# An explicit order for every operation on its engine, in a fused linear-attention and Fourier-mix kernel on one core

## The chip, the core and the metric

The kernel runs on one core of a Trainium2 chip. The metric is the device time of one execution in microseconds (us). The core has five engines with instruction queues of their own, which the profile names PE (TensorE, with PEld for its weight loads), DVE (VectorE), ACT (ScalarE), POOL (GpSimd) and SP (SyncE, which only issues transfers here). Each engine works through its queue in order, and queues wait for each other by semaphores.

## The reference, cut to what matters

Four batches, eight heads, 768 steps of time, 48 channels per head. The first part is a linear attention with a decaying state, the second a Fourier mix and an MLP of 384 to 1536 to 384:

```python
for t in range(S):
    cur = np.einsum('bhd,bhe->bhde', u[None] * kt, vt)
    y[:, :, t] = np.einsum('bhd,bhde->bhe', rt, state + cur)
    state = wt[:, :, :, None] * state + np.einsum('bhd,bhe->bhde', kt, vt)
...
X = np.fft.fft(np.fft.fft(x, axis=1), axis=2)
u = x + np.real(X)
un = (u - mu) / np.sqrt(var + 1e-06)
out = u + np.maximum(un @ w_ch1, 0.0) @ w_ch2
```

## The kernel before

The time axis is cut into chunks of 128 steps: 6 chunks per batch, 24 in all, numbered n. `attention(b, c)` describes one chunk. The logarithm of the decay (`Ln`, tile lb) is summed along time by two matmuls (`tce`, `tci`), exponentials on ScalarE (`ex`, `ew`) make the decays, VectorE and GpSimd multiply them onto r and k (`rh`, `kh`), TensorE transposes both (`trr`, `trk`), the copies `rT` and `kT` bring the transposes from PSUM to SBUF, `am` makes the matrix of scores, VectorE masks it (`ms`, tile ah), `sm` and `st` carry the state on, and `y` makes the result; `rk`, `rku`, `dc`, `vtd` and `yx` add the term with u. In batch 0 `kh` is VectorE's, later GpSimd's, behind the exponential of line 736 (tile e). `fe` and `fo` fold the result for the Fourier sums.

`mix(b)` does the rest of a batch: `sq` (sequence sums, matmuls of 193 columns), `hc` and `hr` (copies), `dm` (sums over the channels), `uf`, `bs`, `ba` (residual, mean and variance), `un`, `tr`, `ut` (normalised, transposed, copied out of PSUM), then layer 1 (`m1`, line 958) with its relu (`rl`) and layer 2 (`m2`, line 974) with `ob` (tile osb) and the transfer out. Before all that, set-up makes the tables of sines and cosines: VectorE computes arguments (line 553 writes them), ScalarE takes sines, loads its table of logarithm and exponential (line 640), VectorE mirrors the tables and TensorE rearranges them (line 679). Unused columns of some tiles are filled with zeros once (line 556).

No loop order decides when an operation runs. Every operation is registered with `op` under a kind and a number, with its engine, its planned duration and what it reads and writes. `schedule` then plays the plan through: at each step it takes, over all engines, the ready operation that can start first, ties broken by the number in `PLAN`, with limits on open PSUM tiles per pool (`caps`: 5 for attention, 4 for the mix, 1 for the fillers). What comes out is a fixed queue per engine. `PLACES` holds a digit for each operation that can run on two engines: 0 ScalarE, 1 VectorE for `rT`, `kT`, `hc`, `ut` and `rl`. Loads keep the order w, k, r, v of each chunk (`o.prev`). `fill_gaps` puts matmuls of zeros, the fillers of line 1015, where the plan leaves TensorE idle, from the first operation `beat` until planned time 56 us; they keep one PSUM bank.

```python
c = (s, o.key, o.idx)
if best is None or c < best[0]:
    best = (c, o)
```

Of the kernel before, what the change touches and what calls it, by code (L numbers as in the profile page):

```python
# [7 lines left out]
ALU = mybir.AluOpType  # L8
# [24 lines left out]
class _Prog:  # L33
# [13 lines left out]
    RATE = 192.0  # L47
    AHEAD = 1500.0
    DMA_LEAD = 500.0

    def __init__(self, nc, caps, plan, places):
        self.nc = nc
        self.ops = []
        self.wr = {}
        self.rd = {}
        self.caps = caps
        self.plan = plan
        self.places = places

# [3 lines left out]
    def op(self, lab, alts, r=(), w=(), sem=None, nbytes=0, fix=0.0):  # L63


        kind, n = lab
# [31 lines left out]
    def schedule(self):  # L98
        free = [0.0] * 8
        users = [()] * 8  # L100
        BUSY = 1e17
        held = {p: 0 for p in self.caps}
        engt = {e: 0.0 for e in self.ENGS}
        avail = {e: [] for e in self.ENGS}
        order = {e: [] for e in self.ENGS}
        dma_t = 0.0
        port_t = 0.0
        for o in self.ops:
            for d in o.deps:
                d.users.append(o)  # L110
            o.nd = len(o.deps)
            o.ready = o.ready0
            if o.nd == 0:
                avail[o.eng].append(o)
        left = len(self.ops)
        while left:
            best = None
            spare = sorted(f for f in free if f < BUSY)
            for e in self.ENGS:
                for o in avail[e]:  # L120
                    if o.prev is not None and o.prev.start is None:
                        continue
                    s = max(engt[e], o.ready)
                    if o.port:
                        s = max(s, port_t)
                    if o.bytes and e == "sp":
                        s = max(s, dma_t - self.AHEAD)
                    if o.opens:
                        new = [x for x in o.tile if x.ops[0] is o]
                        if held[new[0].pool] + len(new) > self.caps[new[0].pool] or len(spare) < len(new):  # L130
                            continue
                        s = max(s, spare[len(new) - 1])
                    c = (s, o.key, o.idx)
                    if best is None or c < best[0]:
                        best = (c, o)
# [3 lines left out]
            avail[e].remove(o)  # L139
            for x in o.tile:  # L140
                if x.ops[0] is o:
                    idle = [i for i in range(8) if free[i] <= s]
                    if idle:
                        x.bank = max(idle, key=lambda i: (free[i ^ 1], -i))
                    else:
                        x.bank = min(range(8), key=lambda i: (free[i], i))
                    o.deps.update(users[x.bank])
                    free[x.bank] = BUSY
                    held[x.pool] += 1
# [9 lines left out]
            order[e].append(o)  # L159
            for x in o.tile:  # L160
                x.n_done += 1
                x.end = max(x.end, o.end)
                if x.n_done == len(x.ops):
                    held[x.pool] -= 1
                    free[x.bank] = x.end + self.BANK_LAT
                    users[x.bank] = tuple(x.ops)
            for u in o.users:
                if o.bytes:
                    t = o.end
                elif e == u.eng == "pe":  # L170
                    t = engt[e]
                else:
                    t = o.end + self.LAT[e][u.eng]
                u.ready = max(u.ready, t)
                u.nd -= 1
                if u.nd == 0:
                    avail[u.eng].append(u)
# [4 lines left out]
    def fill_gaps(self, fn, tile, dur, spare, until):  # L182
# [5 lines left out]
        for o in self.order["pe"]:  # L188
            n = int((o.start - t - spare) // dur) if first.start < o.start <= min(until, last.start) else 0
# [105 lines left out]
    def _topo(self):  # L295
# [3 lines left out]
        while n < len(self.ops):  # L299
# [13 lines left out]

PLAN = {
    "set": [573, -700, -711, -727, -138, 1123, 29, -1164, 314, 1326, 325, -916, -2410, -588, -1687, -469, 1954, -296, 3463,
# [4 lines left out]
    "zero": [2203],  # L320
    "load": [2835, -3063, -2612, -1806, 887, -2150, 635, -954, 767, 394, 1084, -1028, -1889, -641, -923, 248, -88, -1448,
           2009, -1694, -1788, 966, -1289, -1158],
    "Ln": [284, -611, 1645, -1456, -2505, 255, -669, 148, 585, -1351, -1052, -503, -1122, 769, 337, 3689, -172, -915, 688,
           -3266, 412, 3417, -623, -5688],
    "tce": [-1829, -3214, -1237, -1827, -876, 33, -456, -1340, -1828, -2352, 144, 733, -77, -51, -421, 1795, -245, -547, -113,
           -1271, 702, 1074, -434, 693],
    "tci": [1561, -9, -2535, 1234, -298, 3695, -2840, -1446, -1807, -1864, 1253, -2594, 653, -665, -434, -773, 1708, -5099,
           748, -2106, 1377, -22, 669, 128],
    "ex": [-3131, 1004, -188, 739, 237, 1443, -1155, 5815, -1424, -194, 2886, -202, 469, 929, 431, -3017, -1192, -640, -1072,
           -655, 2635, -532, -275, -1379],  # L330
    "tot": [-105, -660, -616, 1383, -1284, 0, -2541, -1074, -1853, -911, -928, 0, 1115, -2238, 147, -601, 792, 0, 96, -1156,
           203, -267, -1607],
# [9 lines left out]
    "vtd": [2161, -2040, -532, -1785, -2577, 377, -865, 1608, 3126, 1151, 2646, -927, 358, -1231, -1689, -3886, -971, -1826,
           -95, -3035, -391, 789, -1252, 795],
    "vb": [-955, -2112, 3388, 415, -509, -390, -277, 132, -715, 1212, 427, 4272, -590, 346, -2779, 390, 792, 158, 2849, 907,
           1735, 830, 58, 3257],
    "rh": [412, 1151, -212, 2002, 243, 179, 159, 1558, -530, -1849, -1998, -751, -415, -500, 247, -1541, 471, 1405, -2535,
           -1777, -1851, -220, 556, -1131],
# [84 lines left out]
def bass_rwkv6_finch__then__fnet_fourier_mix_kernel(  # L432
# [13 lines left out]
    CH = 128  # L446
# [603 lines left out]
```

How the kernel before makes its waits and increments, by code:

```python
        def run(name, eng):  # L259
            for o in self.order[name]:
                for c, v, d in sorted(o.waits, key=lambda x: x[2].end):
                    eng.wait_ge(sems[c], d.val)
                ins = o.fn(eng)
                if o.sem is not None:
                    ins.then_inc(sems[o.sem], 16)
                elif o.inc:
                    ins.then_inc(sems[name], 1)
            if name == "dve":
                for s in dcount:
                    if s.startswith("out"):
                        eng.wait_ge(sems[s], dcount[s])
                eng.nop()
```

## Time and profile before

| | |
|---|---|
| median of 3 runs | 204.85 us (204.56 to 205.8) |
| the profiled execution | 204.85 us, its span 203.1 us |
| TensorE | 190.9 us busy, 1847 matmuls |
| VectorE | 170.4 us busy, 430 instructions |
| ScalarE | 126.6 us busy |
| GpSimd | 109.5 us busy |

The span runs from the first to the last instruction of the profiled execution; the rest of its time lies around that. A busy time is the union of an engine's instruction records. Matmuls are pipelined, so that records of neighbours overlap. "Idle before" is the time for which an engine had nothing in work ahead of an instruction, with what released it.

### The profile page before, as it was taken

How to read it: one execution, taken by the hardware profiler on the slowest of the kernel's cores; microseconds unless marked ns; L12 is line 12 of the kernel's file. 1: busy time of each engine (PE TensorE's matmuls, PEld its weight loads, DVE VectorE, ACT ScalarE, POOL GpSimd, SP SyncE). 2: the span in 40 equal slices, each digit the busy share in tenths (PEclk: the TensorE clock that was granted, in tenths of full speed). 3: DMA queues.
4: the chain of work that ended last, by engine and by line, in shares of the span. 5: the costliest groups of instructions: out<-in, count | busy, mean ns of one | idle time of the engine just before them, and what ended most of it. 6: DMA issues, size and time to landing. Idle time of an engine off the chain costs nothing.

```text
span 203.1 us, 4857 instructions
## 1 busy us (share of the span) xinstructions
PE 190.9 (94%) x1847; PEld 124.0 (61%) x1847; DVE 170.4 (84%) x430; ACT 126.6 (62%) x291; POOL 109.5 (54%) x131
## 2 busy tenths in 40 slices
PE   0999899999999999899899999999999999999993
PEld 0765575766656666666456667666666666666561
DVE  8939997989889899999999999998989769674332
ACT  4589785336757989667989587549872452936000
POOL 2353759741038899999699789992233550000000
PEclk9999999999999999999999999999999999999999
DMA  6999998999999707999999659512001200210033
GB/s 129 193 202 195 198 204 140 200 184 185 195 187 206 160 0 160 215 186 199 268 175 226 137 136 211 122 39 81 0 3 39 81 0 0 84 37 0 0 116 116
DMA packets 105414, 26.45 MB, mean 130 GB/s; under 512 B 100272, under 2 KB 105008, under 8 KB 105392
## 3 DMA queue, kind: packets, MB, share of 16 engines
q1 hardware_dynamic: 103440, 23.80, 55.2%
q0 software_dynamic: 1952, 2.36, 7.0%
q8 instruction: 14, 0.23, 0.4%
q14 instruction: 8, 0.07, 0.1%
HBM read 23.79 MB, written 4.72 MB: 140 GB/s over the span
## 4 chain that ended last, share of the span: by engine, by line
PE 63%; DVE 22%; POOL 7%; ACT 3%; issue 3%; POOLq 0%; DVEq 0%; ACTq 0%
PE bank L958 19%; PE bank L974 19%; PE bank L1015 5%; DVE ah L796 4%; PE bank L887 4%; PE bank L913 3%; POOL rk L545 2%; PE bank L791 2%; DVE st L817 2%; DVE uf L918 2%; POOL kh L545 2%; DVE rh L753 2%; PE bank L931 2%; PE bank L769 2%; DVE bst L921 2%
## 5 line engine op out<-in xcount | busy, mean ns | idle before, releaser
L958 PE MATMUL bank<-unt,w 128*128 128x384 bf16 x288 | 54.2, 326 | 0.8 <-ACT ht L963 0.3
L974 PE MATMUL bank<-w,ht 128*128 128x384 bf16 x288 | 52.5, 326 | 0.3 <-ACT ht L963 0.2
L963 ACT ACTIVATE ht<-bank 128x384 bf16<-128x384 f32 x59 | 28.5, 492 | 13.6 <-PE bank L958 13.3
L974 PEld LDWEIGHTS bank<-w,ht 128*128 128x128 bf16 x288 | 26.6, 98 | 16.2 <-ACT ht L963 0.4
L958 PEld LDWEIGHTS bank<-unt,w 128*128 128x128 bf16 x288 | 25.9, 97 | 16.6 <-ACT ht L963 0.7
L796 DVE TENSOR_TENSOR ah<-bank,msk 128x512 bf16<-128x512 f32 x48 | 31.3, 679 | 1.5 <-PE bank L791 1.3
L545 POOL TENSOR_TENSOR vtd<-in_v,dc 128x384 f32<-128x384 f32 x24 | 19.9, 829 | 18.4 <-DVE dc L744 12.7
L545 POOL TENSOR_TENSOR kh<-in_k,e 128x384 bf16<-128x384 f32 x18 | 18.0, 1002 | 16.3 <-ACT e L736 16.3
L545 POOL TENSOR_TENSOR rk<-in_r,in_k 128x384 f32<-128x384 f32 x24 | 23.9, 1000 | 4.9 <-DMA in_r<-in_r_dram 4.8
L964 DVE TENSOR_SCALAR ht<-bank 128x384 bf16<-128x384 f32 x37 | 19.7, 552 | 7.6 <-PE bank L958 7.4
L545 POOL TENSOR_TENSOR rk<-rk,ub 128x384 f32<-128x384 f32 x24 | 23.9, 999 | 2.5 <-DMA ub<-in_u_dram 1.8
L559 ACT ACTIVATE un<-uf,agg 128x384 bf16<-128x384 f32 x24 | 14.1, 609 | 15.6 <-DVE agg L923 15.4
L980 DVE SCALAR_TENSOR_TENSOR osb<-bank,rstd,uf 128x384 f32<-128x384 f32 x24 | 14.4, 609 | 11.0 <-PE bank L974 10.2
L545 POOL TENSOR_TENSOR xf<-fd,ft 128x384 bf16<-128x384 f32 x18 | 17.7, 1001 | 9.4 <-DVE ft L859 8.4
L1015 PE MATMUL bank<-wz 128*128 128x256 bf16 x105 | 16.6, 297 | 4.8 <-DVE wz L556 4.8
L846 ACT ACTIVATE x<-bank 128x384 f32<-128x384 f32 x24 | 11.8, 490 | 9.8 <-DVE bank L842 5.4
L721 ACT ACTIVATE bank<-bank 128x384 f32<-128x384 f32 x24 | 11.8, 491 | 8.5 <-PE bank L715 8.5
L753 DVE TENSOR_TENSOR rh<-bank,in_r 128x384 bf16<-128x384 f32 x24 | 13.2, 549 | 3.3 <-ACT bank L721 3.2
L817 DVE TENSOR_TENSOR st<-bank,e 64x192 bf16<-64x192 f32 x40 | 14.0, 351 | 1.4 <-PE bank L835 0.8
L1015 PEld LDWEIGHTS bank<-wz 128*128 128x128 bf16 x105 | 10.7, 106 | 7.2 <-DVE wz L556 4.8
L744 DVE TENSOR_REDUCE dc<-rk 128x8 f32<-128x384 f32 x24 | 12.9, 541 | 0.1
L918 DVE TENSOR_TENSOR uf<-bank,x 128x384 f32<-128x384 f32 x24 | 12.6, 545 | 0.2 <-PE bank L913 0.2
(120 smaller groups left out, 373.0 us busy)
## 6 DMA issues: line engine op xcount, KB each, us to landing
in_w<-in_w_dram SPq DMA_DIRECT2D x24, 192.0 KB, 3.9
in_k<-in_k_dram SPq DMA_DIRECT2D x24, 192.0 KB, 4.0
in_r<-in_r_dram SPq DMA_DIRECT2D x24, 192.0 KB, 4.2
in_v<-in_v_dram SPq DMA_DIRECT2D x24, 192.0 KB, 4.0
out_dram<-osb SPq DMA_DIRECT2D x24, 192.0 KB, 1.9
w<-in_moe_w_ch_dram POOLq DMA_DIRECT2D x2, 1152.0 KB, 13.7
ub<-in_u_dram SPq DMA_DIRECT2D x1, 192.0 KB, 4.4
```

The source lines that it names most:

```text
L545: return shared(lambda e: e.tensor_tensor(out=o, in0=a, in1=b, op=f))
L559: return lambda e: e.activation(o, a, f, **kw)
L753: op(("rh", n), ("dve", 551, lambda e: e.tensor_tensor(out=rh[:, :, 0:D], in0=ps(tce)[:, 0:DM].rearrange("t (h d) -> t h d", d=D), in1=rt[ ...
L796: masked[n] = op(("ms", 2 * n + x), ("dve", 682, lambda e, x=x: e.tensor_tensor(out=ah[:, x:H:2, :], in0=ps(ta[x])[:, :].rearrange("p (h t ...
L817: op(("st", 2 * n + x), ("dve", 360, lambda e, x=x, pr=pr: e.tensor_tensor(out=s_out[pr, :, D * x:D * x + D], in0=ps(tds)[pr, 0:DM].rearra ...
L918: op(("uf", n), ("dve", 543, lambda e, kb=kb, t=t: e.tensor_tensor(out=uf[:, kb, :], in0=ps(t)[:, 0:DM], in1=xb[:, kb, 0:DM], op=ALU.add)) ...
L958: ins = e.matmul(ps(t)[:, 0:384], W1[:, m, 128 * j:128 * j + 128], unt[:, m, :], start=(m == 0), stop=(m == NM - 1))
L963: ("act", 490, lambda e, j=j, t=t, ht=ht: e.activation(ht[:, j, :], ps(t)[:, 0:384], ACTF.Relu)),
L964: ("dve", 552, lambda e, j=j, t=t, ht=ht: e.tensor_scalar(out=ht[:, j, :], in0=ps(t)[:, 0:384], scalar1=0.0, scalar2=None, op0=ALU.max))],
L974: ins = e.matmul(ps(t)[:, 0:DM], ht[:, j, 128 * x:128 * x + 128], W2[:, j, :], start=(j == 0), stop=(j == NJ - 1))
L980: op(("ob", n), ("dve", 614, lambda e, kb=kb, t=t, o=o: e.scalar_tensor_tensor(out=o[:, :], in0=ps(t)[:, 0:DM], scalar=rstd[:, kb:kb + 1], ...
L1015: return e.matmul(ps(tw)[:, 0:256], WZ[:, 0:128], WZ[:, :])
```

## The change

The numbers in `PLAN` become places: `schedule` sorts each engine's operations by them and takes only the head of each queue. Its planned times now set nothing but the PSUM bank of a tile and the number of fillers. The limits per pool and the fixed order of loads are gone, and so is the wait of `tce` for the mask of two chunks before. Set-up registers index patterns and fills first, then the tables; a fill may be VectorE's or GpSimd's by a digit in `PLACES`, and two state fills become one. `sq` places pairs of matmuls together. The second `beat`, where the fillers end, now reads what a relu of the first half batch writes. A few planned durations and rates differ.

```diff
-    def __init__(self, nc, caps, plan, places):
+    def __init__(self, nc, plan, places):
...
     def schedule(self):
+        order = {e: sorted((o for o in self.ops if o.eng == e), key=lambda o: o.key) for e in self.ENGS}
+        head = {e: 0 for e in self.ENGS}
...
-            for e in self.ENGS:
-                for o in avail[e]:
-                    if o.prev is not None and o.prev.start is None:
+            for x, e in enumerate(self.ENGS):
+                if head[e] >= len(order[e]):
+                    continue
+                o = order[e][head[e]]
+                if o.nd:
+                    continue
...
-    "zero": [2203],
+    "zero": [51, 7, 15, 8, 11, 38, 40, 42, 3, 2, 10, 15, 9, 50, 5, 46, 4, 8, 18, 41, 6, 7, 1],
...
-    "beat": [-514, 2562],
+    "beat": [113, 118],
...
 PLACES = {
-    "rT": "010000010000010000110111",
-    "kT": "110011011000100111000100",
-    "hc": "110001010000",
-    "ut": "011111000001000010010101",
-    "rl": "101111100000001000000010101000000001000011111000010000100000100110110100111111010010100001111000",
+    "zero": "01011000011100000010100",
+    "rT": "100000110100000010000100",
+    "kT": "010000011100000010011000",
+    "hc": "001000000001",
+    "ut": "100100000000000000000101",
+    "rl": "011100001100010011010000100000100000010000000110000110011001100000101011010000000111010101110010",
 }
...
+    def zeros(ap, dve, pool, w, val=0.0):
+        f = fill(ap, val)
+        op(("zero", 0), [("dve", dve + 35, f), ("pool", pool, f)], w=w)
...
         for i in range(2):
-            put("dve", 145, fill(ST[i][0:64, :, D:2 * D], 0.0), w=[("ST", i, 0)])
-            put("dve", 145, fill(ST[i][64:128, :, 0:D], 0.0), w=[("ST", i, 1)])
+            zeros(ST[i][:, :, :], 223, 480, [("ST", i, 0), ("ST", i, 1)])
...
-        if n >= 2:
-            o.deps.add(masked[n - 2])
...
-    small_constants()
+    iotas()
+    fills()
     tables()
     masks()
-    fills()
     mirrors()
...
-    for i in range(2):
-        o = op(("beat", i), ("pe", 110, beat), r=["WZ"], w=[tw])
-        o.ready0 = WARM * i
+    op(("beat", 0), ("pe", 110, beat), r=["WZ"], w=[tw])
+    op(("beat", 1), ("pe", 110, beat), r=["WARM"], w=[tw])
     g.schedule()
-    g.fill_gaps(beat, tw, 110.0, 150.0, WARM)
+    g.fill_gaps(beat, tw, 110.0, 150.0)
```

TensorE's queue from its start. Lines 1015 and 989 are fillers, 679 and 652 the tables, 715 and 686 `tce`, 719 and 688 `tci`, 725 and 694 `tot`, lb0 and lb1 the logarithms of chunks 0 and 1. Before:

```order
L1015 MATMUL bank0<-wz 128x256 x37
L679 MATMUL bank1<-ss,nidw 128x193
L679 MATMUL bank1<-cs,rev 128x193
L679 MATMUL bank1<-ss,idw 128x191
L679 MATMUL bank1<-cs,rev 128x191
L679 MATMUL bank2<-cs,rev 128x193
L679 MATMUL bank2<-cs,rev 128x191
L679 MATMUL bank3<-ss,nidw 128x193 x2
L679 MATMUL bank3<-ss,idw 128x191 x2
L715 MATMUL bank4<-lb0,msk 128x384
L719 MATMUL bank5<-lb0,nle 128x384
L725 MATMUL bank5<-one,lb0 128x1 x4
```

After:

```order
L652 MATMUL bank0<-ss,nidw 128x193
L652 MATMUL bank0<-cs,rev 128x193
L652 MATMUL bank0<-ss,idw 128x191
L652 MATMUL bank0<-cs,rev 128x191
L652 MATMUL bank1<-cs,rev 128x193
L652 MATMUL bank1<-cs,rev 128x191
L688 MATMUL bank2<-lb1,nle 128x384
L694 MATMUL bank2<-one,lb1 128x1 x4
L652 MATMUL bank3<-ss,nidw 128x193 x2
L652 MATMUL bank3<-ss,idw 128x191 x2
L686 MATMUL bank4<-lb0,msk 128x384
L686 MATMUL bank5<-lb1,msk 128x384
```

The 37 fillers ahead of the tables are gone, and chunk 1's sums stand among the tables. The queue after has a filler in two places only, both amid layer 1 of the first half batch.

VectorE's queue in set-up, where the first steps of the tables stand (ht1 and uf1 are scratch; the first rows before are the end of the fills that begin the queue). Before, the ninth instruction to the first table step:

```order
L556 MEMSET kh0 128x8x8
L556 MEMSET kh2 128x8x8
L556 MEMSET bhpi 128x1
L556 MEMSET lb1 128x8x8
L556 MEMSET beps 128x1
L556 MEMSET xf0 128x6x32
L556 MEMSET lb0 128x256
L550 TENSOR_SCALAR chs<-tc 128x1
L549 TENSOR_SCALAR tn<-tc 128x3
L549 TENSOR_SCALAR msk<-ht1 128x128
L549 TENSOR_SCALAR sgi<-tci 128x1
L550 TENSOR_SCALAR ht1<-ht1,tn 128x194
```

After, the first twelve:

```order
L517 TENSOR_SCALAR tn<-tc 128x3
L524 MEMSET ss 128x3
L517 TENSOR_SCALAR msk<-ht1 128x128
L524 MEMSET kh1 128x8x8
L524 MEMSET xf0 128x6x33
L524 MEMSET st1 128x192
L518 TENSOR_SCALAR ht1<-ht1,tn 128x194
L524 MEMSET cs 128x3
L524 MEMSET x0 128x6x4
L524 MEMSET lb2 128x8x8
L518 TENSOR_SCALAR nle<-ht1 128x128
L518 TENSOR_SCALAR ht1<-ht1 128x194
```

The first step of the tables (`ht1<-ht1,tn`) moves from twentieth to seventh place.

ScalarE's queue where batch 0 reaches the MLP: un is the normalised row, ht the relu, e_1 the exponential on which GpSimd's `kh` of chunk 7 waits. Before:

```order
L559 ACTIVATE un<-uf,agg 128x384
L963 ACTIVATE ht<-bank 128x384
L559 ACTIVATE un<-uf,agg 128x384
L944 ACTIVATE lnv<-agg,beps 128x3
L963 ACTIVATE ht<-bank 128x384
L559 ACTIVATE vb<-in_v 128x384
L947 ACTIVATE rstd<-lnv 128x3
L559 ACTIVATE lb<-in_w 128x8x48
L963 ACTIVATE ht<-bank 128x384
L846 ACTIVATE x<-bank 128x384
L736 ACTIVATE e_1<-bank 128x388
L721 ACTIVATE bank<-bank 128x384
```

After:

```order
L750 ACTIVATE ktb<-bank 128x512
L875 ACTIVATE hcs<-bank 128x2x193 x2
L527 ACTIVATE vb<-in_v 128x384
L527 ACTIVATE un<-uf,agg 128x384 x3
L914 ACTIVATE unt<-bank 128x3x128 x2
L690 ACTIVATE bank<-bank 128x384
L705 ACTIVATE e_1<-bank 128x388
L527 ACTIVATE lb<-in_w 128x8x48
L527 ACTIVATE un<-uf,agg 128x384
L938 ACTIVATE ht<-bank 128x384 x2
L914 ACTIVATE unt<-bank 128x3x128
L938 ACTIVATE ht<-bank 128x384 x2
```

That exponential has moved ahead of the first relu; before, it stood behind four.

The order of the loads changes too: r2, k0, r1, w0, u, w1, k1, r0, w2, w3, r3, k2, v0 are the first thirteen (the digit is the chunk), in place of w0, k0, r0, v0, u, w1, k1, r1, v1, w2, k2, r2, v2.

## Rows read from the trace of the kernel before

**Rows 1.** The page: span, then part 1, busy time, share, instructions.
```profile
span 203.1 us, 4857 instructions
...
PE 190.9 (94%) x1847; PEld 124.0 (61%) x1847; DVE 170.4 (84%) x430; ACT 126.6 (62%) x291; POOL 109.5 (54%) x131
```

**Rows 2.** Stages: length, then busy (x instructions) PE, PEld, DVE, ACT, POOL; clock, DMA.
```profile
10.80:49.80 39.00, 37.03 (x407) 24.47 (x407) 33.02 (x78) 25.18 (x62) 22.69 (x26) 1.00 1.07 191
49.80:140.00 90.20, 87.96 (x926) 57.21 (x927) 85.05 (x200) 68.26 (x158) 72.62 (x81) 1.00 0.77 162
140.00:200.00 60.00, 59.92 (x485) 37.85 (x481) 41.99 (x97) 27.59 (x64) 10.89 (x13) 1.00 0.10 37
```

**Rows 3.** The same view of L1015 alone: PE, PEld; clock, DMA; two calls.
```profile
0.00:10.80 10.80, 5.98 (x37) 4.46 (x37) 1.00 0.81 163
10.80:49.80 39.00, 10.31 (x68) 6.15 (x67) 1.00 1.07 191
...
7.80:8.80 1.00, 1.00 (x7) 0.76 (x6) 1.00 0.93 187
8.80:9.80 1.00, 1.00 (x11) 0.90 (x10) 1.00 1.09 214
```

**Rows 4.** Timeline of PE: start, us, instruction.
```profile
10.78 0.26 PE L679 MATMUL bank<-ss,nidw 64*128 64x193 bf16 x1
```

**Rows 5.** Timeline of DVE, set-up; in brackets the idle time before.
```profile
2.76 0.31 DVE L550 TENSOR_SCALAR ht<-ht,tn 128x194 f32<-128x194 f32 x1
...
5.55 1.16 DVE L553 SCALAR_TENSOR_TENSOR uf<-ht,tc 128x194 f32<-128x194 f32 x1
...
7.50 0.40 DVE L553 SCALAR_TENSOR_TENSOR uf<-ht,tc 128x194 f32<-128x194 f32 x1
...
8.02 0.34 DVE L553 SCALAR_TENSOR_TENSOR ht<-uf 128x194 f32<-128x194 f32 x1
...
13.08 0.56 DVE L753 TENSOR_TENSOR rh<-bank,in_r 128x384 bf16<-128x384 f32 x1 [2.29 <-ACT bank L721]
```

**Rows 6.** Timeline of ACT, set-up.
```profile
8.94 1.28 ACT L640 ACT_TABLE_LOAD   x1
...
10.66 0.51 ACT L559 ACTIVATE lb<-in_w 128x384 bf16<-128x384 f32 x1
```

**Rows 7.** Timeline of POOL, set-up and batch 0 to 1.
```profile
5.50 1.00 POOL L545 TENSOR_TENSOR rk<-in_r,in_k 128x384 f32<-128x384 f32 x1 [3.55 <-DMA in_r<-in_r_dram]
8.29 1.00 POOL L545 TENSOR_TENSOR rk<-rk,ub 128x384 f32<-128x384 f32 x1 [1.80 <-DMA ub<-in_u_dram]
...
31.46 0.93 POOL L690 DMA_DIRECT2D w<-in_moe_w_ch_dram  x1
...
58.05 1.01 POOL L545 TENSOR_TENSOR kh<-in_k,e 128x384 bf16<-128x384 f32 x1 [10.90 <-ACT e L736]
```

**Rows 8.** Timeline of SP, the queue that issues the loads (fifth and thirteenth).
```profile
3.73 0.71 SPq L580 DMA_DIRECT2D ub<-in_u_dram  x1
...
11.62 0.90 SPq L575 DMA_DIRECT2D in_v<-in_v_dram  x1
```

**Rows 9.** The chain that ended last: start, us, what.
```profile
29.57 0.65 PE bank L824 x2
...
49.81 3.59 PE bank L958 x21
...
69.91 0.82 POOL vtd L545
...
177.98 10.24 PE bank L958 x63
```

**Rows 10.** Groups of DVE by form: busy us, mean ns of one, idle before.
```profile
L940 DVE CAST unt<-bank 128x384 bf16<-128x384 f32 x10 | 5.4, 547 | 0.0
L782 DVE COPY ktb<-bank 128x512 bf16<-128x512 bf16 x11 | 4.6, 416 | 0.3 <-PE bank L775 0.3
...
L901 DVE CAST hcs<-bank 128x386 bf16<-128x386 f32 x4 | 2.2, 588 | 0.6 <-PE bank L887 0.6
```

More of the change, by code:

```diff
@@ L55, in __init__ @@
         self.rd = {}
-        self.caps = caps
         self.plan = plan
         self.places = places
+        self.count = {}
     def tile(self, pool):
@@ L63, in op @@
     def op(self, lab, alts, r=(), w=(), sem=None, nbytes=0, fix=0.0):
-        kind, n = lab
+        kind = lab[0]
+        n = self.count.get(kind, 0)
+        self.count[kind] = n + 1
         if isinstance(alts, tuple):
@@ L98, in schedule @@
     def schedule(self):
+        order = {e: sorted((o for o in self.ops if o.eng == e), key=lambda o: o.key) for e in self.ENGS}
+        head = {e: 0 for e in self.ENGS}
+        engt = {e: 0.0 for e in self.ENGS}
+        BUSY = 1e17
         free = [0.0] * 8
         users = [()] * 8
[L101 to L105, printed above, removed]
         dma_t = 0.0
@@ L117, in schedule @@
             best = None
-            spare = sorted(f for f in free if f < BUSY)
-            for e in self.ENGS:
-                for o in avail[e]:
-                    if o.prev is not None and o.prev.start is None:
-                        continue
[L123 to L135, printed above, removed]
+            for x, e in enumerate(self.ENGS):
[4 more added lines that the diff above has]
+                    continue
+                s = max(engt[e], o.ready)
+                if o.opens:
+                    n = sum(t.ops[0] is o for t in o.tile)
+                    spare = sorted(f for f in free if f < BUSY)
+                    if len(spare) < n:
+                        continue
+                    s = max(s, spare[n - 1])
+                a = s
+                if o.bytes and e == "sp":
+                    s = max(s, dma_t - self.AHEAD)
+                if o.port:
+                    s = max(s, port_t)
+                if best is None or (s, a, x) < best[0]:
+                    best = ((s, a, x), o)
             assert best is not None, "no operation can start"
@@ L138, in schedule @@
             e = o.eng
-            avail[e].remove(o)
-            for x in o.tile:
-                if x.ops[0] is o:
+            head[e] += 1
+            for t in o.tile:
+                if t.ops[0] is o:
                     idle = [i for i in range(8) if free[i] <= s]
[L143 to L149, printed above, removed]
+                    t.bank = max(idle, key=lambda i: (free[i ^ 1], -i))
+                    o.deps.update(users[t.bank])
+                    free[t.bank] = BUSY
             o.start = s
@@ L158, in schedule @@
                 o.end = s + o.dur + (self.DRAIN if e == "pe" else 0.0)
[L159 to L166, printed above, removed]
+            for t in o.tile:
+                t.n_done += 1
+                t.end = max(t.end, o.end)
+                if t.n_done == len(t.ops):
+                    free[t.bank] = t.end + self.BANK_LAT
+                    users[t.bank] = tuple(t.ops)
             for u in o.users:
@@ L188, in fill_gaps @@
         for o in self.order["pe"]:
-            n = int((o.start - t - spare) // dur) if first.start < o.start <= min(until, last.start) else 0
+            n = int((o.start - t - spare) // dur) if first.start < o.start <= last.start else 0
             for i in range(n):
@@ L342 @@
[L342 to L347, printed above, removed]
@@ new lines @@
+    "beat": [113, 118],
[23 rows of a table added]
+    "zero": [51, 7, 15, 8, 11, 38, 40, 42, 3, 2, 10, 15, 9, 50, 5, 46, 4, 8, 18, 41, 6, 7, 1],
[19 rows of a table added]
+    "rku": [13, 14, 17, 21, 27, 28, 34, 44, 43, 49, 57, 52, 63, 77, 83, 85, 82, 91, 96, 99, 112, 118, 117, 121],
+    "vtd": [20, 22, 23, 24, 29, 31, 37, 46, 50, 54, 60, 58, 70, 78, 86, 88, 90, 97, 109, 104, 119, 122, 124, 127],
+    "wgt": [30, 40],
[3 rows of a table added]
+    "load": [3, 1, 7, 12, 4, 5, 6, 2, 16, 8, 11, 0, 15, 9, 13, 10, 20, 14, 22, 18, 25, 17, 21, 19, 28, 23, 24, 29, 26, 27, 32,
[3 rows of a table added]
@@ L647, in mirrors @@
             lo = [(n + "l", q) for q in range(NS)]
-            put("dve", 60, fill(T[:, :, 1, HK - 1:HK], 0.0), w=[(n + "x", q) for q in range(NS)])
             put("dve", 303, ts(T[:, :, 0, HQ:HK], T[:, :, 0, HQ - 2::-1], sg[:, :], None, ALU.mult),
```

152 lines of the change are left out of this document (64 added, 88 removed), and 129 rows, old and new, of the table PLAN.

## The prediction

> **What bounds the kernel now.** I read the busy shares first, then the span by stage, and only then single waits, because the shares mislead here. TensorE shows 94% busy and VectorE 84% [rows 1]. By stage [rows 2] VectorE is busy 33.0 of the 39.0 us from 10.8 to 49.8 us and 85.1 of the 90.2 us up to 140 us (94%); after that it falls to 42.0 of 60.0, while TensorE is busy throughout. So VectorE sets the pace until about 140 us, and TensorE the rest. TensorE's 98% in the middle stage overstates it: records of matmuls overlap, and 63 matmuls of 384 columns really take 10.24 us, 163 ns each [rows 9].
>
> Part of TensorE's busy time is no work at all: fillers (matmuls of zeros, L1015) take 5.98 us before 10.8 us and 10.31 us of the stage behind it [rows 3]. Real work starts at 10.78 us because the tables aren't there earlier [rows 4]. VectorE makes their arguments, and its first product of the attention (rh) starts at 13.08 us after an idle 2.29 us [rows 5]. The chain to there: the last argument at 8.02 us on VectorE [rows 5], ScalarE's sine of it, the table load at 8.94 us, the logarithm (lb) at 10.66 us [rows 6]. The MLP's first layer (L958) starts at 49.81 us [rows 9].
>
> **The change part by part.** All sums go against the profiled execution: 204.85 us, of which 203.1 us is the span [rows 1] and 1.75 us lies around it. The median of the runs shown is the same 204.85.
>
> *Set-up, -2.0 us.* Before, fifteen fills stand ahead of the tables on VectorE and the first table step starts at 2.76 us [rows 5]. Now two small set-up steps and four fills do, and it can start near 2.1 us: 0.65 us. Between first and last argument fills, sign columns and the second identity leave (about 1.2 us of start-to-start time) and four small ones come (0.5 us): 0.7 us. One step took 1.16 us, its sister 0.40 [rows 5]: it ran beside GpSimd's rk of 5.50 us [rows 7]. That rk now waits for k1, the seventh load, and stays clear: 0.76 us. So the last argument comes 2.1 us earlier and the table load ends near 8.1 us. There the loads become the limit, w1 being the sixth now. The fifth (ub), issued at 3.73 us [rows 8], had landed by 8.29 us [rows 7]; from it to the thirteenth issue at 11.62 us [rows 8] it is 0.99 us a load, so w1 lands near 9.2 us. Then a logarithm of 0.51 [rows 6], a matmul and its wait, about 0.35, and two exponentials in a queue on ScalarE, about 0.9: rh at about 11.0 instead of 13.08 us. Bounds: -3 us (w1 comes sooner) to +1 us (GpSimd's fills are slow and loads late). The v0 load falls from fourth to thirteenth place: 11.62 + 4.56 (ub's time) = 16.2 us. TensorE's queue holds its first reader, the state matmul, and what stands behind that; VectorE has ten other operations until then. I count 0, at worst 1 us.
>
> The eight fills on GpSimd lie in its idle 3.55 us ahead of rk [rows 7]: 0, at worst half a microsecond for those ahead of the tables' index pattern.
> The Trainium skill speaks against it: "SBUF — State Buffer", section "Who interferes with whom", says that GpSimd and VectorE share a port pair, and that a tensor_scalar in a two-port mode and a GpSimd operation shut each other out. By that a fill beside a table step can hold it up; with half a microsecond for it (an estimate) the whole would be 199.9 us. The 1.16 us row agrees that the two collide; no run here shows a GpSimd fill doing it.
>
> *Batch 0, -2.5 us.* Copies out of PSUM move from VectorE to ScalarE: in batch 0 three kT, one hc and three ut leave, one relu comes. At 416, 588 and 547 ns [rows 10], the relu priced as ut, that is 1.25 + 0.59 + 1.64 - 0.55 = 2.9 us; neighbours overlap by some 0.08 us each, so 2.5. VectorE's idle time in 10.8 to 49.8 us is 6.0 us, 2.3 of it the wait for the first rh, so 3.7 us of slack: I count all of the 2.5. Bounds: -4 (waits shrink too) to 0 (ScalarE, busy 25.2 of 39.0 us [rows 2], answers later).
>
> *Batches 1 and 2, -2.5 us.* Two hc, two ut, two kT and one relu leave VectorE, two rT come: 1.18 + 1.09 + 0.83 + 0.55 - 0.83 = 2.8 us, net 2.4, in the stage where VectorE is 94% busy. By its records TensorE can give only 2.2 us there, by its spacing more. A second effect: GpSimd idled 10.90 us until 58.05 us, waiting for the exponential e [rows 7], and from 69.91 us it carries the longest chain [rows 9]. The changed order puts that exponential ahead of the MLP's first relu, so kh comes some 10 us earlier. I count 2.5 us for both, between 0 (TensorE full) and 5. Batch 3's moves lie where TensorE sets the pace: 0. W1's transfer stood behind vtd of chunk 4, issued at 31.46 us [rows 7], and still does: 0. W2 now stands behind kh of chunk 7; most of layer 1 covers it; if not, up to 3 us.
>
> *Fillers, +1.5 us.* 103 of 105 go; the two left stand inside layer 1. Fillers number 7 in the microsecond from 7.8 us and 11 in the next [rows 3]: TensorE goes from its lower level, 1.2 GHz, to 2.4 GHz there, after some four microseconds of fillers back to back, though the column of the granted clock prints 1.00. Now the tables meet a TensorE that has done nothing. One chunk's chain through it is 2688 columns (1.14 us at 163 ns per 384) and yx, 0.65 [rows 9]: 1.8 us, at the low level as much again. I take 1.5 for the first chunk, as the wait for v0 hides a little. Bounds: -1.5 us (a filler of 0.11 us less ahead of some dozen real matmuls) to the first rival.
> The skill's page "TensorE: Matmul & The Clock Gate", Part 1, says that the slow level is the default and that activity releases it; the rows above agree. By it batch 0 begins slowly and stays so while TensorE does little, which is the first rival.
>
> Sum: -2.0 - 2.5 - 2.5 + 1.5 = -5.5; 204.85 - 5.5 = 199.35, so **199.4 us**. The tail, one osb and its transfer behind the last matmul, stays.
>
> **The rivals.** (A, slower) *TensorE stays at 1.2 GHz through batch 0.* For: before, only fillers are seen to raise the clock. Against: at half speed the work is twice as dense. Price: per chunk 4352 columns (1.84 us) and yx 0.65, times six 15.0; sequence mixing 48 x 193 columns 3.9, model mixing 18 x 0.163 = 2.9, transposes 0.5: 22.3 us. Doubled, begun at 8.8 us, and with 3.7 us of waits it ends at 57.1, 7.3 us behind 49.81: 204.85 + 7.3 - 2.5 = **209.7 us**. It is slower than before once more than about 17.5 of the 22.3 us run low.
> (B, no change) *GpSimd holds the middle.* For: it is busy 72.6 of 90.2 us [rows 2], carries the chain from 70 us, and its work is the same. Then head and batch 0 only wait in front of it, the fillers' cost is hidden with them, and batches 1 and 2 give 1.2: **203.7 us**. Against: its idle 10.9 us just before. That *the order doesn't do what it says* belongs here: it is frozen from planned times, and if loads land 2 us later than counted, TensorE stands at v0 with all behind it and the head's gain is gone twice: 199.4 + 2.0 + 2.0 = 203.4.
> (C, much faster) *The clock costs nothing and GpSimd's early start pays in full:* 204.85 - 2.0 - 2.5 - 5.0 = **195.4 us**.
>
> **How the numbers follow.** Forecast 0.54, A 0.14, B with the frozen order 0.16, C 0.16. A measurement here can tell about 1%, 2 us, from no change. The forecast's own range, 197 to 202.5, and C are faster: 0.70. B, and a little of A, is within 1%, 202.8 to 206.9: 0.17. The rest of A is slower: 0.13. The range reaches past C and over half of A: 194.5 to 207.5.
>
> **What would show it.** Right: last argument near 6 us, first rh near 11, the first matmul of layer 1 near 46 to 48, kh of chunk 7 ten microseconds earlier, VectorE's total down by some 9 us, the first 384-column matmuls about 320 ns apart and soon 163. Wrong: the wide spacing into batch 0's mixing (A); an early head but the same stage from 70 us on (B); TensorE waiting for v0 or W2.

## Result and the profile after

The changed kernel takes 198.51 us (median of 4 runs, 198.09 to 199.0) against 204.81 us beside it; the ratio is 0.9685, 95% interval 0.965 to 0.9721. In a second series it took 197.97 us (6 runs) against 205.09, ratio 0.9663 (0.9636 to 0.969). So it is 6.3 to 7.1 us faster; 199.4 was forecast, with a range of 194.5 to 207.5.

The page of the changed kernel: span, busy shares, granted clock, chain by engine.

```profile
span 196.7 us, 4656 instructions
...
PE 178.9 (91%) x1744; PEld 117.1 (60%) x1744; DVE 161.9 (82%) x403; ACT 133.2 (68%) x308; POOL 110.9 (56%) x139
...
PEclk9999699999999999999999999999999999999999
...
PE 73%; DMA 7%; DVE 6%; issue 5%; POOL 4%; ACT 4%; DVEq 0%; POOLq 0%; ACTq 0%
```

Against [rows 1] VectorE has 8.5 us less to do, ScalarE 6.6 more and GpSimd 1.4 more. TensorE is busy 12 us less, though 16.3 us of fillers went [rows 3]: the fillers' records overlap those of real matmuls by 3.8 us, and the real matmuls alone cover 178.1 us before and 178.9 us after. Transfers hold 7% of the chain in this execution. In the trace of after_again (the second series) they hold none:

```profile
PE 83%; DVE 9%; ACT 4%; issue 2%; POOL 0%; DVEq 0%; POOLq 0%; ACTq 0%
```

By stage, to be read beside [rows 2] (the borders are the first table, the first matmul of layer 1, 140 us as there, and the end of TensorE's work):

```profile
8.40:46.60 38.20, 33.17 (x357) 21.82 (x357) 32.40 (x80) 29.07 (x68) 23.25 (x30) 0.96 1.00 193
46.60:140.00 93.40, 92.14 (x969) 61.16 (x965) 86.81 (x207) 74.72 (x177) 73.53 (x82) 1.00 0.81 164
140.00:193.00 53.00, 53.00 (x424) 33.97 (x423) 35.63 (x79) 24.40 (x58) 12.54 (x15) 1.00 0.11 39
```

VectorE's share in the middle is 93%, nearly what it was (94%). What fell is its rest behind 140 us, from 42.0 to 35.6 us. About 2.8 us of that (an estimate from the rows of copies) are batch 3's own copies, of which a net six went to ScalarE; most of the rest must have been done earlier.

VectorE's timeline in the set-up, and its last instruction:

```profile
2.14 0.20 DVE L518 TENSOR_SCALAR ht<-ht,tn 128x194 f32<-128x194 f32 x1
...
5.47 0.41 DVE L521 SCALAR_TENSOR_TENSOR uf<-ht,tc 128x194 f32<-128x194 f32 x1
...
6.13 0.35 DVE L521 SCALAR_TENSOR_TENSOR ht<-uf 128x194 f32<-128x194 f32 x1
...
11.92 0.56 DVE L722 TENSOR_TENSOR rh<-bank,in_r 128x384 bf16<-128x384 f32 x1 [3.50 <-ACT bank L690]
...
193.68 0.62 DVE L955 SCALAR_TENSOR_TENSOR osb<-bank,rstd,uf 128x384 f32<-128x384 f32 x1 [0.68 <-PE bank L949]
```

Before, the last instruction stood 6.34 us later:

```profile
200.02 0.62 DVE L980 SCALAR_TENSOR_TENSOR osb<-bank,rstd,uf 128x384 f32<-128x384 f32 x1 [0.68 <-PE bank L974]
```

ScalarE in the set-up:

```profile
7.07 1.28 ACT L614 ACT_TABLE_LOAD   x1
8.68 0.94 ACT L527 ACTIVATE lb<-in_w 128x384 bf16<-128x384 f32 x2 [0.32 <-DMA in_w<-in_w_dram]
...
11.31 0.47 ACT L690 ACTIVATE bank<-bank 128x384 f32<-128x384 f32 x1 [0.51 <-PE bank L686]
```

The tables' last argument comes 1.9 us earlier than in [rows 5], the step that took 1.16 us takes 0.41, and the logarithm (lb) comes 2.0 us earlier than in [rows 6]. From lb to the first rh, though, it is 3.24 us where it was 2.42, and VectorE idles 3.50 us in front of it. TensorE's timeline says why, and shows two later places:

```profile
10.75 0.85 PE L686 MATMUL bank<-lb,msk 128*128 128x384 bf16 x2
11.39 0.53 PE L688 MATMUL bank<-lb,nle 128*128 128x384 bf16 x1
...
20.49 1.49 PE L793 MATMUL bank<-vtd,ht 128*128 128x384 f32 x2
...
27.44 0.83 PE L793 MATMUL bank<-vtd,ht 128*128 128x384 f32 x2
...
46.80 0.65 PE L933 MATMUL bank<-unt,w 128*128 128x384 bf16 x3
...
61.75 0.81 PE L949 MATMUL bank<-w,ht 128*128 128x384 bf16 x4 [1.00 <-DMA w<-in_moe_w_ch_dram]
```

At 10.75 us two matmuls of 384 columns take 0.64 us from start to the next start, 320 ns each: 1.2 GHz, although the clock's column prints 1.00 there. The pair of matmuls of yx at 20.49 us is slow again, 1.49 us where a later one takes 0.83. Layer 1 begins at 46.80 us (before: 49.81 [rows 9]), and layer 2 waits 1.00 us for its weights W2 at 61.75 us. GpSimd's timeline belongs to that:

```profile
33.87 0.93 POOL L663 DMA_DIRECT2D w<-in_moe_w_ch_dram  x1
...
47.53 1.00 POOL L513 TENSOR_TENSOR kh<-in_k,e 128x384 bf16<-128x384 f32 x1 [4.10 <-ACT e L705]
48.47 1.07 POOL L664 DMA_DIRECT2D w<-in_moe_w_ch_dram  x1
```

kh of chunk 7 stands at 47.53 us in place of 58.05 [rows 7], with 4.10 us of idle time ahead of it in place of 10.90. W2 is issued behind it. VectorE's groups by form, for [rows 10]:

```profile
L751 DVE COPY ktb<-bank 128x512 bf16<-128x512 bf16 x7 | 2.9, 417 | 0.9 <-PE bank L744 0.9
L751 DVE COPY rtb<-bank 128x512 bf16<-128x512 bf16 x6 | 2.5, 411 | 0.1
L915 DVE CAST unt<-bank 128x384 bf16<-128x384 f32 x4 | 2.2, 552 | 0.8 <-PE bank L906 0.8
L876 DVE CAST hcs<-bank 128x386 bf16<-128x386 f32 x2 | 1.2, 598 | 2.1 <-PE bank L858 2.1
```

Four kT, two rT, six ut and two hc copies and three relus have left VectorE on balance; each of the copies that stayed costs what it did.

### The profile page after: what moved, and what is told of

The parts are those of the page before. It is cut to its first block, busy times and chain, and to the rows that moved or that the text cites. A ratio compares the mean times of both kernels' runs of the same rounds, so it can differ in the third digit from the quotient of the medians.

```text
span 196.7 us, 4656 instructions
## 1 busy us (share of the span) xinstructions
PE 178.9 (91%) x1744; PEld 117.1 (60%) x1744; DVE 161.9 (82%) x403; ACT 133.2 (68%) x308; POOL 110.9 (56%) x139
## 4 chain that ended last, share of the span: by engine, by line
PE 73%; DMA 7%; DVE 6%; issue 5%; POOL 4%; ACT 4%; DVEq 0%; POOLq 0%; ACTq 0%
PE bank L949 24%; PE bank L933 19%; DMA w<-in_moe_w_ch_dram 7%; PE bank L888 4%; PE bank L858 3%; PE bank L744 3%; PE bank L760 3%; PE bank L738 2%; PE bank L688 2%; PE bank L804 2%; PE bank L686 2%; PE bank L906 2%; PE bank L801 1%; PE bank L793 1%; PE bank L778 1%
## 5 line engine op out<-in xcount | busy, mean ns | idle before, releaser
L949 PE MATMUL bank<-w,ht 128*128 128x384 bf16 x288 | 55.5, 326 | 1.0 <-DMA w<-in_moe_w_ch_dram 1.0
L938 ACT ACTIVATE ht<-bank 128x384 bf16<-128x384 f32 x62 | 29.3, 492 | 17.6 <-PE bank L933 14.3
L939 DVE TENSOR_SCALAR ht<-bank 128x384 bf16<-128x384 f32 x34 | 18.3, 548 | 8.3 <-PE bank L933 8.2
L527 ACT ACTIVATE lb<-in_w 128x384 bf16<-128x384 f32 x24 | 12.5, 526 | 0.3 <-DMA in_w<-in_w_dram 0.3
L896 DVE BATCH_NORM_STATS2 bst<-uf 128x6 f32<-128x384 f32 x24 | 12.6, 545 | 0.1
```

Source lines behind the costliest of these rows:

```text
L527: return lambda e: e.activation(o, a, f, **kw)
L938: ("act", 490, lambda e, j=j, t=t, ht=ht: e.activation(ht[:, j, :], ps(t)[:, 0:384], ACTF.Relu)),
L939: ("dve", 552, lambda e, j=j, t=t, ht=ht: e.tensor_scalar(out=ht[:, j, :], in0=ps(t)[:, 0:384], scalar1=0.0, scalar2=None, op0=ALU.max))],
L949: ins = e.matmul(ps(t)[:, 0:DM], ht[:, j, 128 * x:128 * x + 128], W2[:, j, :], start=(j == 0), stop=(j == NJ - 1))
```

## Experiments

Ratios are to the kernel before, run beside each. The changed kernel stands at 0.9685 and 0.9663, so differences under about 0.7 us from it are not told apart; where a difference in us to it is given, it is (ratio - 0.967) x 205.

**The set-up.** All 23 fills on VectorE, 22 of them first:

```diff
-    "zero": [51, 7, 15, 8, 11, 38, 40, 42, 3, 2, 10, 15, 9, 50, 5, 46, 4, 8, 18, 41, 6, 7, 1],
+    "zero": [50, -30, -29, -28, -27, -26, -25, -24, -23, -22, -21, -20, -19, -18, -17, -16, -15, -14, -13, -12, -11, -10, -9],
...
-    "zero": "01011000011100000010100",
+    "zero": "00000000000000000000000",
```

> The changed kernel with all its constant fills on VectorE and 22 of them ahead of the tables, as the kernel before had it; nothing else moves. T (the head start of the set-up is kept to the end): the last table argument comes at about 8 us in place of 6.13, the first rh at 13 to 13.5, and the time rises by 1.0 to 1.9 us to 199.5 to 200.4. Rival (the start is absorbed by the first batch, whose chunks wait for other things): 198.1 to 198.9.

Measured: 199.0 us, ratio 0.9712 (0.9674 to 0.975): 0.9 us up, too near the interval to count. VectorE's timeline shows that the start moves as a whole:

```profile
7.16 0.35 DVE L521 SCALAR_TENSOR_TENSOR ht<-uf 128x194 f32<-128x194 f32 x1
...
12.92 0.56 DVE L722 TENSOR_TENSOR rh<-bank,in_r 128x384 bf16<-128x384 f32 x1 [3.55 <-ACT bank L690]
```

Last argument and first rh are both 1.0 us later than in the changed kernel (the trace is of the slowest of four runs, 200.65 us). So the places of the fills are worth 1.0 us at the head, about half of the 2.06 us that the set-up gains there when TensorE is not slow (fillers_head, below).

**The fillers.** Three kernels. The first puts 46 fillers back ahead of the tables, the second has them in TensorE's gaps as well, and the third takes 103 out of the kernel before.

```diff
# fillers_head
-    "beat": [113, 118],
+    "beat": [-2, -1],
...
-    "zero": [51, 7, 15,
+    "zero": [-1, 7, 15,
...
-    op(("beat", 1), ("pe", 110, beat), r=["WARM"], w=[tw])
+    op(("beat", 1), ("pe", 110, beat), r=["NIDW"], w=[tw])
-    g.fill_gaps(beat, tw, 110.0, 150.0)
+    g.fill_gaps(beat, tw, 165.0, 150.0)
# fillers_through: the same, but
+    "beat": [-1, 118],
...
     op(("beat", 1), ("pe", 110, beat), r=["WARM"], w=[tw])
# before_no_fillers
-    g.fill_gaps(beat, tw, 110.0, 150.0, WARM)
+    g.fill_gaps(beat, tw, 110.0, 150.0, 0.0)
```

> The changed kernel with 46 filler matmuls put back, all of them ahead of the first table matmul, as in the kernel before; nothing else moves. T (the low clock of the first chunk is a price that still stands in the new order): TensorE is at 2.4 GHz from about the first table matmul on, the tables and the first 384-column matmuls take half as long, the first rh comes at about 11.0 us in place of 11.92, there is no low stretch at 20.7 to 24.1, and the time falls by 1.0 to 1.5 us, to about 197.3. Rival (the low clock is hidden beside VectorE and ScalarE, which have the set-up to do): 198.1 to 198.9, no change. Second rival (the fillers delay the tables, being in front of them on TensorE): over 199.

> The changed kernel with fillers ahead of the tables as in fillers_head, and now also in TensorE's gaps of the first chunks, as the kernel before had them. fillers_head measured a ratio of 0.9643 against before where the changed kernel had 0.9685, and in its trace the clock was granted in full for only 6.8 us and was then at 1.2 GHz for 10.2 us, over the gap in front of chunk 0. T (that second low stretch costs about as much as the first saved): TensorE stays at 2.4 GHz from the tables on, the first rh comes at about 11.0, the first layer-1 matmul a further 0.5 to 1 us earlier than in fillers_head, and the time is 0.5 to 1.0 us under it, about 197. Rival (after the first rh the chunks wait for VectorE and GpSimd, and the clock is covered): as fillers_head, within 0.3 us.

> The kernel before with 103 of its 105 fillers left out and nothing else changed. T: it pays what the prediction put on the fillers, 1.5 us: TensorE stays at 1.2 GHz until about 17 us, the first rh comes 0.3 to 1 us later than 13.08, and the time is about 206.3. Rival (fillers are only in the way, and the low clock is hidden): 204.8 or up to 1 us less.

fillers_head: 197.84 us, 0.9643 (0.962 to 0.9665), 0.6 us down, not told apart from nothing. In its trace the first rh comes at 11.02 us, 0.90 earlier, as theory T had it; but TensorE falls back at once. Its timeline:

```profile
10.05 0.49 PE L686 MATMUL bank<-lb,msk 128*128 128x384 bf16 x2
...
13.15 1.07 PE L744 MATMUL bank<-idw,kh 128*128 128x128 bf16 x8 [2.37 <-DVE kh L726]
...
14.33 0.85 PE L688 MATMUL bank<-lb,nle 128*128 128x384 bf16 x2
```

The pair of 384-column matmuls takes 0.49 us ahead of the wait of 2.37 us and 0.85 behind it. The 0.90 us last for a while: layer 1 starts 0.93 us earlier than in the changed kernel (45.87 against 46.80).

```profile
45.87 2.11 PE L933 MATMUL bank<-unt,w 128*128 128x384 bf16 x12
```

Behind that the two executions come together. The wait for W2 is 1.4 us in this one and 1.0 in the other, and the last osb is 0.13 us earlier (193.55 against 193.68).

fillers_through: 199.05 us, 0.9708 (0.9677 to 0.974), 0.8 us up; T falls. In its trace the first table matmuls take 0.26 us each, as in fillers_head (0.34 in the changed kernel), no low stretch follows, and the first rh comes at 10.90 us. Yet nothing is gained: layer 1 starts at 47.62 us, 1.75 later than in fillers_head, where T had it earlier. ScalarE's start times, laid side by side with those of the changed kernel, are 1.28 us ahead at 14 us, 0.94 at 27, 0.18 at 32, and 0.82 behind at 46. One place can be read in TensorE's timeline: two fillers stand at 27.69 us ahead of yx, with no idle time beside them, and TensorE, 0.84 us ahead until then, is 0.43 ahead behind them. That fillers in gaps of the plan that are none in the run did the rest too is likely, but not shown place by place. As its fillers hold the queue up, this kernel can't say what a full clock alone would be worth at the end.

before_no_fillers: 1.0063 (1.0032 to 1.0094), 1.3 us slower, the size that T had; but the place seems to be another. Its twelve runs fall into three groups: four with a mean clock of 1.00 took 205.2 to 205.5 us, no more than before; five with 0.992 took 207.0 to 207.2; three with 0.982 or 0.983 took 208.1 to 208.6. The first rh comes at 13.24 us (before: 13.08). The trace is of one of the last three (208.3 us). It has a low stretch around the first matmuls of layer 1, behind three microseconds in which TensorE is busy 1.16:

```profile
47.00:50.00 3.00, 1.16 (x9) 0.58 (x9) 3.00 (x10) 1.95 (x5) 0.00 (x0) 0.83 1.26 204
50.00:53.00 3.00, 2.37 (x9) 1.19 (x9) 2.39 (x6) 1.33 (x3) 0.00 (x0) 0.50 0.97 194
```

So in the old order the fillers bought nothing at the first chunk that shows. That they paid ahead of layer 1 is what this one trace suggests; where the other runs had their low stretches is not known, so it is not shown.

**Copies against order.** 85 of the 180 copies out of PSUM (rT, kT, hc, ut and the relus) change engine, 51 from VectorE to ScalarE and 34 back: 17 net. In each of these four kernels the order is planned as it was, the copies named change engine, and every engine's list is then sorted by planned start; the other instructions keep their order, but for a filler here and there. The PSUM banks of the tiles are planned anew along with it, and what that does is not parted from what the engines do. The core of the edit in the changed kernel:

```diff
+        keep = [set(o.deps) for o in self.ops]
+        self.play({e: sorted((o for o in self.ops if o.eng == e), key=lambda o: o.key) for e in self.ENGS})
+        for o, d in zip(self.ops, keep):
...
+            if o.lab[0] in OLD:
+                o.eng, o.dur, o.fn = o.alts[int(OLD[o.lab[0]][o.idx0])]
...
+        self.play({e: sorted((o for o in self.ops if o.eng == e), key=lambda o: o.start) for e in self.ENGS})
```

> The changed kernel's order, with the rT, kT, hc, ut and rl copies put back on the engine (VectorE or ScalarE) that they had in the kernel before, each at its planned place in time; TensorE's and GpSimd's orders and the set-up stay as in the changed kernel. T (the gain behind the set-up comes from the work taken off VectorE): loses 4 to 4.5 of the 6.3 us, about 202.8, VectorE busy about 8 us more. Rival (the order alone makes the gain, and where a copy runs is worth little): within 1 us of 198.5.

> The kernel before, in its own scheduler's order, with the rT, kT, hc, ut and rl copies put on the engines that they have in the changed kernel, each at its planned place in time; set-up, fills and fillers stay as before, GpSimd's order is the same. T (work taken off VectorE is the gain): VectorE is busy some 8 us less than 170.4, and the time falls by 3 to 5 us, to about 201. Rival (the copies' engines are worth nothing without the new order): 204 to 206, no change or slightly worse, the old order being made for the old places. old_places measured the other corner: 205.8, no gain left with the new order and the old places.

> The changed kernel's order with only 17 copies put back from ScalarE to VectorE at their planned places (2 rT, 4 kT, 2 hc, 6 ut, 3 rl, spread over the program), which is the whole net shift of copies between the two engines; old_places put back all 85 that changed engine (51 one way, 34 the other) and measured 205.8. Load theory (17 copies' worth of time on VectorE is the gain): VectorE as busy as in old_places, 168, and nearly the same time, 204 to 206. Fit theory (each order is made for its own places, and each copy on the other engine costs where it stands): about 17 of the 85 misfits, a rise of 1 to 2 us over the changed kernel, 199.5 to 201.

> The kernel before in its own order with 17 copies moved from VectorE to ScalarE at their planned places (2 rT, 4 kT, 2 hc, 6 ut, 3 rl), the net shift of the change and nothing else; before_new_places, with all 85, measured 210.8. Load theory: VectorE's busy time falls by about 8 us and the time by 2 to 4 us, to 201 to 203. Fit theory: no gain, 205 to 207, the copies being late or in the way on ScalarE where they now stand.

| order | all 85 on the other kernel's engine | the net 17 alone |
|---|---|---|
| new | old_places 205.8, 1.0023 (1.0004 to 1.0042) | net_back 202.72, 0.9882 (0.9854 to 0.991) |
| old | before_new_places 210.82, 1.0275 (1.024 to 1.0309) | before_net 205.26, 1.0009 (0.9991 to 1.0027) |

Busy shares and chain of net_back:

```profile
PE 181.8 (91%) x1744; PEld 117.6 (59%) x1744; DVE 168.4 (84%) x420; ACT 126.7 (63%) x291; POOL 111.0 (55%) x139
...
PE 58%; DVE 36%; issue 3%; ACT 2%; POOL 0%; DVEq 0%; POOLq 0%; ACTq 0%
```

and of before_net:

```profile
PE 191.7 (94%) x1847; PEld 124.5 (61%) x1847; DVE 165.3 (81%) x413; ACT 133.2 (65%) x308; POOL 110.1 (54%) x131
...
PE 62%; DVE 22%; ACT 12%; issue 2%; DVEq 0%; ACTq 0%
```

with the chain of the kernel before for it:

```profile
PE 63%; DVE 22%; POOL 7%; ACT 3%; issue 3%; POOLq 0%; DVEq 0%; ACTq 0%
```

In the new order 17 copies back on VectorE give it 6.5 us more work, the end comes 4.3 us later, and VectorE's share of the chain rises from 6% or 9% (the two traces of the changed kernel) to 36%: here VectorE's load is on the path. In the old order the same shift takes 5.1 us off VectorE, gives ScalarE 6.6 us more, and the time doesn't move. With all 85, VectorE has 3.9 us less to do (166.5) and the kernel is 5.8 us slower. In the new order too the load is not all: old_places has the same 168.4 us on VectorE as net_back and is 2.9 us slower. So neither theory holds by itself. The load theory had the right direction in the new order, but forecast 204 to 206 for net_back, and it fails in the old order; the fit theory was right on before_net and priced net_back two to four times too low. Each of these kernels changes ScalarE's work by as much as VectorE's or more, so none of them parts the two; that it is VectorE's load which counts in the new order is read from the chain alone.

Part of net_back's loss may be the clock's. In its trace 384-column matmuls are slow up to 22.59 us and fast at 25.92, while in the changed kernel's trace the clock was granted in full from 17.3 to 20.7 us. Its layer 1 starts at 49.24 us, 2.44 later than in the changed kernel, from the same first rh (11.92):

```profile
22.59 0.48 PE L702 MATMUL bank<-lb,msk 128*128 128x384 bf16 x1 [0.21 <-DVE dc L729]
...
25.92 0.33 PE L704 MATMUL bank<-lb,nle 128*128 128x384 bf16 x1
...
49.24 2.11 PE L949 MATMUL bank<-unt,w 128*128 128x384 bf16 x12 [0.64 <-ACT lb L543]
```

fills_first, slow as long and with no copy moved, falls back 0.7 us against the changed kernel over the same stretch. So some 1.7 of the 2.44 us are left for the copies (an estimate).

The Trainium skill, "Perfetto Trace Analysis", section "Optimizing Scalar/DVE Operations", says that moving work to ScalarE may make sense where VectorE is saturated. VectorE looks saturated in both kernels (94% and 93% of the middle stage); net_back agrees with the page; in before_net the move gains nothing.

**GpSimd.** The kernel before, where GpSimd's product for the u-term has 128x1x2 elements from chunk 6 on (it leaves out most of that term):

```diff
-        op(("rku", n), product(rk[:, :, :], rk[:, :, :], UB[:, :, :], ALU.mult, 1000),
+        few = (slice(None), slice(0, 1 if n >= NC else H), slice(0, 2 if n >= NC else D))
+        op(("rku", n), product(rk[few], rk[few], UB[few], ALU.mult, 1000),
```

> The kernel before, in the same order on every engine, with GpSimd's product for the u-term cut to 128x1x2 elements from chunk 6 on; it leaves out most of that term in these chunks, about 16 us of GpSimd's work from 50 us on. Rival B of the prediction (GpSimd holds the middle): TensorE's waits between 60 and 140 us go and the time falls by 3 us or more, to 202 or less. T (VectorE and its share of copies hold it): falls by less than 1 us.

Measured: 205.06 us, 1.0007 (0.9984 to 1.0031). Its stage from 60 to 140 us, and below it the same of the kernel before:

```profile
60.00:140.00 80.00, 78.03 (x843) 50.88 (x842) 76.51 (x180) 61.36 (x142) 57.99 (x79) 1.00 0.74 158
```

```profile
60.00:140.00 80.00, 78.03 (x842) 50.80 (x840) 76.47 (x180) 61.41 (x142) 70.68 (x80) 1.00 0.75 160
```

GpSimd has 12.7 us less to do there, and the busy times of the other engines stay the same. So GpSimd's load does not hold the middle, though its vtd stood in the longest chain [rows 9], and rival B is out.

**W2 and the loads.**

```diff
-    "wgt": [30, 40],
+    "wgt": [30, 30.5],
```

> The changed kernel with the second weight load issued by GpSimd right behind the first, ahead of kh of chunk 6, instead of behind kh of chunk 7; all else keeps its order. T (TensorE's 1.0 us wait for these weights at 61.75 is on the path): the wait goes and the time falls by 0.5 to 1.0 us against the changed kernel. Rival (the wait is covered by the work that TensorE would wait for next, or the earlier transfer takes time from the chunk loads): within 0.3 us, or slower.

> The changed kernel itself, once more, beside head_and_w2 on the same chip, to have differences under 1 us from one chip. Every theory: 198.0 to 199.0 and a ratio of 0.966 to 0.971 to the kernel before.

w2_early: 198.75 us, 0.9683 (0.9648 to 0.9717): no gain. The 1.00 us wait is gone from its trace, and that execution took 197.62 us; but the trace of after_again, the changed kernel once more (197.69 us), has no such wait either. So the wait belongs to some executions only (fills_first has one of 1.3 us), and this pair can't say what an earlier W2 is worth where the wait occurs.

> The changed kernel with the fillers of fillers_head and the early second weight load of w2_early together, as a version that may beat both kernels. Two gains that add (0.85 us and the 1.0 us wait that went from TensorE's path in w2_early's trace): 196.7 to 197.4. Rival (each is taken back by what stands behind it): 198 to 199, as the changed kernel.

head_and_w2: 198.59 us, 0.968 (0.9654 to 0.9707), so the two don't add. Its chain holds a chunk's load of w, and ScalarE waits for it:

```profile
34.67 17.53 DMA in_w<-in_w_dram
...
52.23 0.52 ACT L527 ACTIVATE lb<-in_w 128x384 bf16<-128x384 f32 x1 [1.97 <-DMA in_w<-in_w_dram]
```

The load lands at 52.20 us, and TensorE waits 2.0 us for what ScalarE does behind it. The transfers are busy throughout here: the DMA share is 1.00 up to 46.6 us in the changed kernel. That W2, going first, made this load late is likely, but not shown.

## Why the prediction was right, step by step

*Set-up, -2.0: right, but the low clock took 0.90 of it back.* The first table step stands at 2.14 us (2.1 was worked out), the last argument at 6.13 (8.02 - 2.1 = 5.9). rh came at 11.92, 1.16 us earlier in place of 2.0. With TensorE at 2.4 GHz (fillers_head) it comes at 11.02, 2.06 earlier, as the sum had it. So the difference is the clock's. That the sum fits is partly luck: w1 was there by 8.6 to 8.7, not 9.2, and from there to rh it takes 2.4 us in fillers_head, not the 1.8 that were worked out.
The fills left ahead of the first table step cost little: it starts where it was forecast. The step that took 1.16 us takes 0.41 with GpSimd's rk out of its way. The half microsecond that was worked out beside the Trainium skill's "SBUF — State Buffer", section "Who interferes with whom", was not paid; GpSimd's fills ran before 2.3 and after 10.3 us, so only the first table step could meet one, and it took 0.20 us. msk, ahead of it, took 0.38 us beside GpSimd's work where it had taken 0.22, so at most 0.16 us was paid. (The step of 1.16 us is a scalar_tensor_tensor, not the tensor_scalar of the sentence that the prediction set it beside.)

*Batch 0, -2.5: 1.85.* From first rh to layer 1 it was 36.73 us and is 34.88. net_back, with six of the copies back in batch 0, starts layer 1 later by 2.44 us, of which some 1.7 are left when the clock's part is taken off: so the copies can carry it.

*Fillers, +1.5: wrong in size.* This is the step that failed. It took 1.5 us for the first chunk and carried them to the end. At the head the cost is 0.90 us (11.92 against 11.02), and it reaches layer 1 (0.93). At the end fillers_head is 0.6 us faster, with an interval that reaches the changed kernel's: 0 to 0.6 us are left. Rival A is out: in the changed kernel's trace TensorE left the low level by about 17 us, and only a stretch from 20.7 to 24.1 us was low again.

The three terms up to layer 1 make -3.0; measured -3.01 (49.81 to 46.80), as -2.06, -1.85 and +0.90. That the sum fits so well is partly luck: two terms are smaller than forecast.

*Batches 1 and 2, -2.5: 3.3.* The last osb comes 6.34 us earlier, 3.3 of them behind the start of layer 1, with 1.0 us lost to W2 in that execution; the mechanism was right and the size low. Behind the start of layer 1 net_back's trace loses 1.6 us against the changed kernel's, and 2.6 against after_again's, which has no wait for W2; so the copies explain about half. The rest is left to the earlier e and kh of chunk 7 and to the order. No run here holds e back alone, so that part is argued, not shown; in after_again's trace GpSimd holds 0% of the chain. For W2 the prediction had up to 3 us if it was not covered: it came to 1.0 us in one execution of the changed kernel and to 0 in another.

*What bounded the kernel before.* "VectorE sets the pace until about 140 us" was wrong as it stood: before_net took 5.1 us off VectorE and light_before 12.7 us off GpSimd, and neither moved the end. So taking work off VectorE by giving it to ScalarE gains nothing in the old order, and GpSimd's load alone doesn't set the pace. What did set it there, the runs don't single out; the chain passes from engine to engine, and with the copies moved ScalarE's share of it went from 3% to 12%. VectorE's load with ScalarE's left as it was, ScalarE's load and TensorE's real matmuls were not tested there. The 4.9 us that the prediction put on copies come out near what net_back measures (4.3 us), but only in the new order: there VectorE's time counts.

## What to carry to other kernels

Work moved off an engine that is 94% busy need not gain anything: with a fixed order on each engine, move a little of its work and see whether the end moves, before pricing a shift of work by its busy time. Places and order belong together: here each of them, put into the other kernel, lost all of the gain or more, so plan both at once and don't carry half of a plan over. Fillers meant to keep a clock up can hold up real work: look in the trace, and not in the plan, whether the queue is idle where they stand.

## What was not expected of the hardware

TensorE's clock falls back in the middle of work. In the changed kernel it was granted in full from about 17.3 us and at half from 20.7 to 24.1 us, and the traces of after_again and w2_early show the same fall; before the fall TensorE had worked 1.80 of 3.30 us, with a wait of 1.10 us among it:

```profile
17.30:20.60 3.30, 1.80 (x26) 1.10 (x27) 2.45 (x7) 3.27 (x9) 2.94 (x4) 1.00 1.00 196
20.80:24.00 3.20, 3.18 (x17) 1.57 (x17) 3.20 (x7) 3.19 (x9) 1.04 (x2) 0.50 1.08 213
```

What that stretch cost is not shown, and the mean clock of a run can't tell. The clock's column prints 1.00 until the first change, so that a low level at the start is not counted. fills_first has a mean clock of 1.00 in its trace, and still its matmuls of 384 columns are slow up to 24 us:

```profile
23.63 0.48 PE L686 MATMUL bank<-lb,msk 128*128 128x384 bf16 x1
...
26.61 0.33 PE L688 MATMUL bank<-lb,nle 128*128 128x384 bf16 x1
```

So a mean clock of 1.00 can stand for an execution that was at 1.2 GHz longer than the changed kernel's trace. In the second series the runs with 1.00 took 198.7 and 198.9 us and those with 0.974 to 0.998 took 197.5 to 198.0; what the low clock costs can't be read from that.
